# A routed expert layer whose first rows come in three transfers, and whose row numbers are moved later

## The chip, the cores and the metric

The kernel runs on one core of one Trainium2 chip. The metric is device time in microseconds (us) of one execution. All engines named here belong to that core: TensorE (PE), VectorE (DVE), ScalarE (ACT), GpSimd (POOL) and SyncE (SP), with 16 DMA engines that all queues share.

## The reference

Three steps follow one another, all in 32-bit floats. First an attention with a decaying state over 768 positions gives 3072 tokens of 384 channels. Then each token goes to the one of 8 experts that its logits pick. Then every token goes through one dense layer pair.

```
x = attention(r, k, v, w, u)                      # (3072, 384)
logits = x @ w_gate; e = argmax(logits)           # one of 8 experts
x[e] = gate * (relu(x[e] @ w1[e]) @ w2[e])        # 384 -> 1024 -> 384
h = x @ w_in; out = max(0.01 * h, h) @ w_out      # 384 -> 2048 -> 384
```

## The kernel before

**Routing.** While the attention runs, POOL scatters finished rows, each of 384 channels and a 385th column with the token's own number, into `x_rows` in DRAM, where every expert has its own region. When the last tile is routed, DVE works out a table of groups: each group is 416 rows of one expert. In the profiled execution there are 8 groups. `grouped` is the semaphore that says the tables are there.

**One group (stage of the experts).** `load_x(n)` (ACT's DMA queue, L1199) brings the 416 rows of group n as 104 partitions x 4 rows x 385 numbers. PE turns them with 12 transposes (L1081), three tiles of columns `d` by four blocks. ACT copies each tile to `x_hi` (L1215), rounded to the matmul's format, and DVE takes the rest, `x_lo` (L1274). Each of 8 hidden blocks `f` is 9 matmuls (L1098: 3 tiles by hi*hi, lo*hi, hi*lo), then a relu by ACT into `h_hi` (L1220) and its rest by DVE into `h_lo` (L1281). Each block goes into the output through 9 more matmuls (L1114), two blocks behind the hidden ones: PE's order in a group is 12 transposes, output blocks 6 and 7 of the group before, hidden 0, 1, 2, output 0, hidden 3, output 1, and so on. The first hidden matmul waits for `parts_ready` of the group's w1, and output block 0 for that of its w2.

**ACT's order in a group.** Three `x_hi` copies, `load_x(n + 1)`, `move_ids(n)`, then the eight relus. `move_ids(n)` (L1208) copies the 416 token numbers of the group, 4 bytes each, from column 385 of `x_rows` to `id_rows` in DRAM. Both read their addresses from the group tables with register loads (L998).

**Weights.** SP loads an expert's weights in seven pieces (three of w1 with 128 x 1024 numbers, four of w2 with 128 x 768) into a `stage` of two halves (L116). Piece m is issued when the split of piece m-2 is done. POOL splits each piece into `w_hi` (L130) and `w_lo` (L134), and small `tick` instructions (L120) carry its waits in the loop. Group 0's weights are ready before the stage begins. The pieces of group 1 are issued once the first rows have landed (SP waits for `x_loaded`). The pieces of w_in and w_out follow those of the last group.

**After the groups.** DVE splits the first dense input (L1297, L1300), PE goes through six dense groups (L1153, L1174), and POOL scatters the results by the numbers from `id_rows`.

Of the kernel before, what the change touches and what calls it, by code (L numbers as in the profile page):

```python
# [13 lines left out]
def build_program(nc, r, k, v, wu, moe_w_gate, moe_w1, moe_w2, moe2_w_in, moe2_w_out, out):  # L14
    C, HP, _, DH, B, P = r.shape
# [9 lines left out]
    DC = D // P  # L25
# [11 lines left out]
    U = 416  # L37
    TR = U // 4
# [8 lines left out]
    x_rows = nc.dram_tensor("x_rows", (E * RR, XW), F32, kind="Internal").ap()  # L47
    id_rows = nc.dram_tensor("id_rows", (N + U, 1), F32, kind="Internal").ap()

    def expert_pieces(e):  # L50
        w1e = moe_w1[e:e + 1] if isinstance(e, int) else moe_w1[bass.ds(e, 1)]
        w2e = moe_w2[e:e + 1] if isinstance(e, int) else moe_w2[bass.ds(e, 1)]
        p = [(c * FE, FE, w1e[:, c * P:(c + 1) * P, :].rearrange("o p f -> p o f")) for c in range(DC)]
        p += [(DC * FE + f * D, 2 * D, w2e[:, f * P:(f + 2) * P, :].rearrange("o (f p) d -> p (o f) d", p=P))
              for f in range(0, FC, 2)]
        return p
# [15 lines left out]
    with ctx:  # L72
        def sb(name, shape, dt=F32, stack=ctx):
            return stack.enter_context(nc.sbuf_tensor(name, shape, dt))
# [4 lines left out]
        def sem(name, stack=ctx):  # L79
            return stack.enter_context(nc.semaphore(name))  # L80
# [858 lines left out]
        def layers():  # L939
# [3 lines left out]
            rows = sb("rows", [P, G, XW], stack=st2)  # L943
# [14 lines left out]
            ps_o = bank[2:6]  # L958


            x_loaded = sem("x_loaded")
            ids_moved = sem("ids_moved")
            xt_mm = sem("xt_mm")
# [32 lines left out]
            def entry(eng, table, n, most):  # L996
                at = table[0:1, n:n + 1] if isinstance(n, int) else table[0:1, bass.ds(n, 1)]
                return eng.value_load(at, min_val=0, max_val=most)  # L998

            def on_sync(sp):  # L1000
                def weights(n, b):
                    e = entry(sp, group_e, n, E - 1)
                    for i, piece in enumerate(expert_pieces(e)):
                        issue_piece(sp, n * NPE + i, (b * NPE + i) % 2, piece)

                sp.wait_ge(grouped, 1)
                pairs, last = pairs_of(sp), last_of(sp)


                sp.wait_ge(x_loaded, 16)  # L1010
                weights(1, 1)
                with sp.Fori(1, pairs) as t:
                    for b in range(2):
                        weights(t * 2 + b, b)
                base = last * NPE + NPE
                for n, piece in enumerate(w_in_pieces()):
                    issue_piece(sp, base + n, n % 2, piece)
                base = base + NPI
                for n, piece in enumerate(w_out_pieces()):
                    issue_piece(sp, base + n, n % 2, piece)  # L1020

                sp.wait_ge(stored, STORES * NG)
# [52 lines left out]
            def on_tensor(pe):  # L1075
                def transposes(n):

                    pe.wait_ge(x_loaded, n * 16 + 16)
                    for d in range(DC):
                        for t in range(4):  # L1080
                            i = pe.transpose(ps_x[d][:, t * TR:(t + 1) * TR], rows[0:TR, t, d * P:(d + 1) * P],  # L1081
                                             ident[0:TR, 0:TR])
                        i.then_inc(xt_mm, 1)
# [47 lines left out]
                pairs, last = pairs_of(pe), last_of(pe)  # L1131
# [61 lines left out]
            def on_scalar(act):  # L1193
                def load_x(n):
                    row = entry(act, group_row, n, E * RR - U)
                    if isinstance(n, int) and n == 0:
                        act.wait_ge(filled, 16 * ZEROS)
                        act.wait_ge(scattered, SCATTERS * C)
                    act.dma_start(rows[0:TR, :, :],  # L1199
                                  x_rows[bass.ds(row, U), :].rearrange("(t p) d -> p t d", p=TR)).then_inc(x_loaded, 16)  # L1200

                def move_ids(n):


                    row, off = entry(act, group_row, n, E * RR - U), entry(act, group_off, n, N)
                    if not isinstance(n, int) or n > 0:
                        act.wait_ge(ids_moved, n * 16)
                    act.dma_start(id_rows[bass.ds(off, U), :], x_rows[bass.ds(row, U), D:D + 1],  # L1208
                                  allow_slow_non_contiguous=True).then_inc(ids_moved, 16)

                def group(n, b):
                    for d in range(DC):

                        act.wait_ge(xt_mm, n * DC + (d + 1))
                        act.activation(x_hi[:, b, d, 0:U], ps_x[d][:, 0:U], ACT.Copy).then_inc(xt_hi_ok, 1)  # L1215
                    load_x(n + 1)
                    move_ids(n)
                    for f in range(FC):
                        act.wait_ge(h_mm, n * FC + (f + 1))
                        act.activation(h_hi[:, f % NB, 0:U], ps_h[f % 2][:, 0:U], ACT.Relu).then_inc(h_hi_ok, 1)  # L1220

                act.wait_ge(grouped, 1)
                pairs = pairs_of(act)
                load_x(0)
                group(0, 0)
                group(1, 1)
                with act.Fori(1, pairs) as t:
                    group(t * 2, 0)
                    group(t * 2 + 1, 1)

                act.wait_ge(ids_moved, pairs * 32)
                act.dma_start(ids_f[:, :].unsqueeze(2), id_rows[U:N + U, :].rearrange("(m p) o -> p m o", p=P),
                              allow_slow_non_contiguous=True).then_inc(ids_in, 16)

                def dense(g, first=False):
                    for f in range(FFC + 1):
                        if f < FFC:

                            act.wait_ge(d_mm, g * FFC + (f + 1))
                            act.activation(hc[:, f % 2, :], ps_h[f % 2][:, :], ACT.Copy).then_inc(d_ok, 1)  # L1240
                        if f >= 1:

                            act.wait_ge(g_ok, g * FFC + f)
                            act.activation(h_hi[:, (f - 1) % NB, :], gf[:, (f - 1) % 2, :], ACT.Copy).then_inc(gh_ok, 1)  # L1244
                    if first:

                        act.wait_ge(x_loaded, pairs * 32 + 16)
                    else:

                        act.wait_ge(stored, g * STORES)  # L1250
                    for t in range(2):
                        act.wait_ge(o_mm, g * G + (t + 1))
                        act.activation(rows[:, t, 0:D], ps_o[t][:, 0:D], ACT.Copy).then_inc(o_act, 1)  # L1253

                dense(0, True)
                with act.Fori(1, NG) as g:
                    dense(g)

            def on_vector(dve):
# [26 lines left out]
                pairs, last = pairs_of(dve), last_of(dve)  # L1286
# [21 lines left out]
                def dense(g, b, more=True):  # L1308
                    for f in range(FFC):

                        dve.wait_ge(d_ok, g * FFC + (f + 1))
                        if not (isinstance(g, int) and g == 0 and f < 2):
                            dve.wait_ge(gh_ok, g * FFC + (f - 1))

                        dve.scalar_tensor_tensor(gf[:, f % 2, :], ps_h[f % 2][:, :], 0.01, hc[:, f % 2, :],  # L1315
                                                 ALU.mult, ALU.max).then_inc(g_ok, 1)
                        dve.wait_ge(gh_ok, g * FFC + (f + 1))
                        dve.tensor_tensor(h_lo[:, f % NB, :], gf[:, f % 2, :], h_hi[:, f % NB, :].bitcast(F32),  # L1318
                                          ALU.subtract).then_inc(gl_ok, 1)
                        if more and f == MID:  # L1320
                            x_split(g + 1, 1 - b)
                        if isinstance(g, int) and g == 0 and f == MID:

                            dve.wait_ge(ids_in, 16)
                            dve.tensor_copy(ids_i[:, :], ids_f[:, :]).then_inc(ids_ok, 1)
                    if not (isinstance(g, int) and g == 0):
                        dve.wait_ge(stored, g * STORES)
                    else:
                        dve.wait_ge(x_loaded, pairs * 32 + 16)
                    for t in range(2, G):  # L1330
                        dve.wait_ge(o_mm, g * G + (t + 1))
                        dve.tensor_copy(rows[:, t, 0:D], ps_o[t][:, 0:D]).then_inc(o_dve, 1)
# [68 lines left out]
```

## Time and profile before

| | us |
|---|---|
| median of 3 runs | 831.3 |
| lowest, highest | 830.53, 842.6 |
| profiled execution, its own time | 825.21 |
| span of the profiled execution | 823.5 |
| PE busy | 771.5 (94%) |
| DVE, ACT, POOL busy | 335.7, 215.1, 335.3 |

The span is what the trace covers, and all places in it below are counted from its start. The attention and the routing end at about 164 us, the groups run from 166 to about 403 us, and the dense layers fill the rest.

### The profile page before, as it was taken

To read this page: it belongs to the slowest core of one execution; us is meant where nothing else is said; L and a number is where in the kernel's file an instruction comes from. 1 tells how busy PE (TensorE), PEld (TensorE's weight loads), DVE (VectorE), ACT (ScalarE), POOL (GpSimd) and SP (SyncE) were. 2 spreads that over 40 slices of the span, in tenths; PEclk is the share of its full clock that TensorE was granted. 3 is DMA by queue.
4 is the path that set the end of the run, shared out by engine and by line. 5 is a ranking of instruction groups with operands and counts; after the bars stand their busy time and mean duration, and the time that the engine had idled before them with its cause. 6 is when DMAs were issued, how large, how long until landed. Compare 5 with 4: busy or idle time off the path is not lost.

```text
span 823.5 us, 17748 instructions
## 1 busy us (share of the span) xinstructions
PE 771.5 (94%) x7200; PEld 707.7 (86%) x7200; DVE 335.7 (41%) x658; ACT 215.1 (26%) x436; POOL 335.3 (41%) x338
## 2 busy tenths in 40 slices
PE   9889889469998989999899999999999999999995
PEld 8778777459998989999889889989988998998994
DVE  7868755613233133223544333433433433433332
ACT  2224433311122112111122232222232223232221
POOL 6568855637767677976991010010010001001001
PEclk9999989779999999999999999999999999999998
DMA  4757654354665355356430000010000000001000
GB/s 145 225 159 208 182 164 148 117 125 136 109 124 150 91 146 157 103 146 146 115 117 1 1 38 1 1 39 1 1 38 0 0 0 38 0 0 39 1 1 39
DMA packets 42611, 66.91 MB, mean 81 GB/s; under 512 B 11413, under 2 KB 31797, under 8 KB 42549
## 3 DMA queue, kind: packets, MB, share of 16 engines
q1 hardware_dynamic: 28944, 50.76, 22.6%
q10 hardware_dynamic: 10533, 5.80, 3.7%
q0 software_dynamic: 3072, 9.45, 3.1%
q8 instruction: 47, 0.77, 0.4%
q14 instruction: 15, 0.12, 0.1%
HBM read 51.42 MB, written 14.59 MB: 80 GB/s over the span
## 4 chain that ended last, share of the span: by engine, by line
PE 79%; POOL 9%; issue 5%; DMA 3%; DVE 2%; ACT 0%; ACTq 0%; POOLq 0%; SPq 0%; DVEq 0%
PE bank L1174 24%; PE bank L1153 24%; PE bank L1114 7%; PE bank L1098 7%; POOL w_lo L134 5%; PE ps_y L833 3%; POOL w_hi L130 2%; DMA stage<-in_moe_w 2%; PE ps_y L818 2%; PE ps_x L790 2%; PE ps_s L770 2%; PE ps_x L786 2%; PE ps_l L854 1%; PE ps_x L845 1%; PE ps_m L804 1%
## 5 line engine op out<-in xcount | busy, mean ns | idle before, releaser
L1042 POOL DMA_INDIRECT out_rows<-rows,ids_i x24 | 23.1, 962 | 358.7 <-ACT rows L1253 353.2
L1318 DVE TENSOR_TENSOR h_lo<-gf,h_hi 128x512 fp32r<-128x512 f32 x96 | 70.2, 732 | 227.4 <-ACT h_hi L1244 227.4
L134 POOL TENSOR_TENSOR w_lo<-stage,w_hi 128x768 fp32r<-128x768 f32 (+1 forms) x70 | 146.4, 2092 | 5.8
L1174 PE MATMUL bank<-w_hi,h_hi 128*128 128x384 f32 x384 | 130.4, 339 | 0.0
L1174 PE MATMUL bank<-w_lo,h_hi 128*128 128x384 f32 x384 | 129.3, 337 | 0.0
L1174 PE MATMUL bank<-w_hi,h_lo 128*128 128x384 f32 x384 | 129.1, 336 | 0.0
L1240 ACT ACTIVATE hc<-bank 128x512 f32<-128x512 f32 x96 | 57.4, 597 | 273.1 <-PE bank L1153 273.1
L1153 PE MATMUL bank<-x_hi,w_hi 128*128 128x512 f32 x288 | 114.0, 396 | 2.3 <-DVE x_lo L1300 2.3
L1153 PE MATMUL bank<-x_lo,w_hi 128*128 128x512 f32 x288 | 114.3, 397 | 0.0
L1153 PE MATMUL bank<-x_hi,w_lo 128*128 128x512 f32 x288 | 113.9, 395 | 0.0
L1281 DVE SCALAR_TENSOR_TENSOR h_lo<-bank,h_hi 128x416 fp32r<-128x416 f32 x64 | 37.7, 591 | 149.5 <-ACT h_hi L1220 149.5
L1220 ACT ACTIVATE h_hi<-bank 128x416 fp32r<-128x416 f32 x64 | 33.0, 517 | 174.2 <-PE bank L1098 170.7
L1174 PEld LDWEIGHTS bank<-w_hi,h_hi 128*128 128x128 f32 x384 | 72.1, 188 | 6.9 <-issue 3.3
L1174 PEld LDWEIGHTS bank<-w_hi,h_lo 128*128 128x128 f32 x384 | 72.2, 188 | 3.5
L130 POOL TENSOR_SCALAR w_hi<-stage 128x768 fp32r<-128x768 f32 (+1 forms) x70 | 65.4, 934 | 20.3 <-DMA stage<-in_moe_w 20.1
L1114 PE MATMUL bank<-h_hi,w_hi 128*128 128x416 f32 x192 | 68.4, 356 | 4.5 <-POOLq L140 4.5
L1174 PEld LDWEIGHTS bank<-w_lo,h_hi 128*128 128x128 f32 x384 | 72.2, 188 | 0.0
L1315 DVE SCALAR_TENSOR_TENSOR gf<-bank,hc 128x512 f32<-128x512 f32 x96 | 65.6, 683 | 11.2 <-ACT hc L1240 11.2
L1098 PE MATMUL bank<-x_hi,w_hi 128*128 128x416 f32 x192 | 68.0, 354 | 0.8 <-DVE h_lo L1281 0.8
L1114 PE MATMUL bank<-h_lo,w_hi 128*128 128x416 f32 x192 | 67.7, 353 | 0.0
L1098 PE MATMUL bank<-x_hi,w_lo 128*128 128x416 f32 x192 | 67.7, 352 | 0.0
L1114 PE MATMUL bank<-h_hi,w_lo 128*128 128x416 f32 x192 | 67.6, 352 | 0.0
(170 smaller groups left out, 1185.5 us busy)
## 6 DMA issues: line engine op xcount, KB each, us to landing
stage<-in_moe_w SPq DMA_DIRECT2D x24, 512.0 KB, 6.0
stage<-in_moe_w SPq DMA_DIRECT2D x32, 384.0 KB, 3.1
rows<-x_rows ACTq DMA_DIRECT2D x9, 625.6 KB
x_rows<-pad_row SPq DMA_DIRECT2D x32, 156.4 KB
k_u<-in_k SPq DMA_DIRECT2D x48, 96.0 KB, 3.0
r_u<-in_r SPq DMA_DIRECT2D x48, 96.0 KB, 2.7
v_u<-in_v SPq DMA_DIRECT2D x24, 192.0 KB, 3.5
stage<-in_moe_w_in SPq DMA_DIRECT2D x6, 512.0 KB, 4.3
```

The costliest lines, as they stand in the source:

```text
L130: eng.tensor_scalar(w_hi[:, buf, off:off + cols], stage[:, h, 0:cols], 1.0, 0.0, ALU.mult, ALU.add).then_inc(split_hi, 1)
L134: i = eng.tensor_tensor(w_lo[:, buf, off:off + cols], stage[:, h, 0:cols], w_hi[:, buf, off:off + cols].bitcast(F32), ALU.subtract)
L833: ins = pe.matmul(ps_y[halves[j], t, b * L:(b + 1) * L], am[halves[j], g % 2, t, b, :], v_cols(i, j, t, b, L), start=False, stop=True, ski ...
L1098: i = pe.matmul(ps_h[f % 2][:, 0:U], ww[:, b, o:o + P], x[:, b, d, 0:U], start=d == 0 and ww is w_hi and x is x_hi, stop=d == DC - 1 and x ...
L1114: i = pe.matmul(ps_y[d][:, 0:U], ww[:, b, o:o + P], h[:, f % NB, 0:U], start=f == 0 and ww is w_hi and h is h_hi, stop=f == FC - 1 and h i ...
L1153: i = pe.matmul(ps_h[f % 2][:, :], ww[:, 0, o:o + P], x[:, b, d, :], start=d == 0 and ww is w_hi and x is x_hi, stop=d == DC - 1 and x is ...
L1174: i = pe.matmul(ps_o[t][:, 0:D], x[:, f % NB, t * P:(t + 1) * P], ww[:, 1, o:o + D], start=f == 0 and x is h_hi and ww is w_hi, stop=f == ...
L1220: act.activation(h_hi[:, f % NB, 0:U], ps_h[f % 2][:, 0:U], ACT.Relu).then_inc(h_hi_ok, 1)
L1240: act.activation(hc[:, f % 2, :], ps_h[f % 2][:, :], ACT.Copy).then_inc(d_ok, 1)
L1281: dve.scalar_tensor_tensor(h_lo[:, f % NB, 0:U], ps_h[f % 2][:, 0:U], 0.0, h_hi[:, f % NB, 0:U].bitcast(F32), ALU.max, ALU.subtract).then_ ...
L1315: dve.scalar_tensor_tensor(gf[:, f % 2, :], ps_h[f % 2][:, :], 0.01, hc[:, f % 2, :], ALU.mult, ALU.max).then_inc(g_ok, 1)
L1318: dve.tensor_tensor(h_lo[:, f % NB, :], gf[:, f % 2, :], h_hi[:, f % NB, :].bitcast(F32), ALU.subtract).then_inc(gl_ok, 1)
```

## The change

The load of group 0 becomes three DMAs, one for each tile of 128 columns, each with its own semaphore `x_first[d]`; the number column isn't loaded for this group. The four transposes of tile `d` wait for `x_first[d]` alone. SP waits for the last of the three. All later loads stay whole, and their counts on `x_loaded` are one load lower. In every group `move_ids(n)` goes from ahead of the relus to behind the second of them.

```diff
@@ on_sync
-                sp.wait_ge(x_loaded, 16)
+                sp.wait_ge(x_first[DC - 1], 16)
                 weights(1, 1)
@@ on_tensor, transposes(n)
-                    pe.wait_ge(x_loaded, n * 16 + 16)
+                    if not isinstance(n, int) or n > 0:
+                        pe.wait_ge(x_loaded, n * 16)
                     for d in range(DC):
+                        if isinstance(n, int) and n == 0:
+                            pe.wait_ge(x_first[d], 16)
                         for t in range(4):
@@ on_scalar, load_x(n)
-                    act.dma_start(rows[0:TR, :, :],
-                                  x_rows[bass.ds(row, U), :].rearrange("(t p) d -> p t d", p=TR)).then_inc(x_loaded, 16)
+                        for d in range(DC):
+                            cols = slice(d * P, (d + 1) * P)
+                            act.dma_start(rows[0:TR, :, cols], x_rows[bass.ds(row, U), cols]
+                                          .rearrange("(t p) d -> p t d", p=TR)).then_inc(x_first[d], 16)
+                    else:
+                        act.dma_start(rows[0:TR, :, :], x_rows[bass.ds(row, U), :]
+                                      .rearrange("(t p) d -> p t d", p=TR)).then_inc(x_loaded, 16)
@@ on_scalar, group(n, b)
                     load_x(n + 1)
-                    move_ids(n)
                     for f in range(FC):
+                        if f == 2:
+                            move_ids(n)
                         act.wait_ge(h_mm, n * FC + (f + 1))
                         act.activation(h_hi[:, f % NB, 0:U], ps_h[f % 2][:, 0:U], ACT.Relu).then_inc(h_hi_ok, 1)
```

ACT's instructions from the first load on stand so before:

```order
L1199 DMA rows<-x_rows 104x4x385
L1215 ACTIVATE x_hi<-bank 128x416 [waits xt_mm] x3
...
L1199 DMA rows<-x_rows 104x4x385
...
L1208 DMA id_rows<-x_rows 416x1
L1220 ACTIVATE h_hi<-bank 128x416 [waits h_mm] x8
```

and so after the change:

```order
L1206 DMA rows<-x_rows 104x4x128
L1206 ISA
L1206 DMA rows<-x_rows 104x4x128
L1206 ISA
L1206 DMA rows<-x_rows 104x4x128
L1225 ACTIVATE x_hi<-bank 128x416 [waits xt_mm] x3
...
L1209 DMA rows<-x_rows 104x4x385
L1231 ACTIVATE h_hi<-bank 128x416 [waits h_mm] x2
...
L1218 DMA id_rows<-x_rows 416x1
L1231 ACTIVATE h_hi<-bank 128x416 [waits h_mm] x6
```

The copy of the numbers and the register loads in front of it moved from ahead of eight relus to between the second and the third.

## Rows read from the trace of the kernel before

**Rows 1.** The page: busy time, and TensorE's clock in 40 slices.

```profile
PE 771.5 (94%) x7200; PEld 707.7 (86%) x7200; DVE 335.7 (41%) x658; ACT 215.1 (26%) x436; POOL 335.3 (41%) x338
PEclk9999989779999999999999999999999999999998
```

**Rows 2.** The chain that ended last: start, length, what.

```profile
165.89 5.88 DMA rows<-x_rows
...
180.08 8.15 DMA stage<-in_moe_w
...
299.79 0.46 PE bank L1114
```

**Rows 3.** Stretches of one group each: length, busy times, clock, DMA share, GB/s.

```profile
199.80:227.80 28.00, 28.00 (x159) 27.94 (x157) 8.02 (x14) 5.47 (x11) 20.93 (x20) 1.00 0.64 136
...
256.00:288.00 32.00, 29.89 (x159) 29.35 (x158) 8.05 (x14) 5.47 (x11) 21.96 (x24) 0.95 0.51 119
288.00:319.30 31.30, 28.95 (x160) 27.94 (x159) 8.04 (x14) 5.47 (x11) 25.88 (x27) 1.00 0.47 134
319.30:347.30 28.00, 28.00 (x159) 27.95 (x158) 8.04 (x14) 5.47 (x11) 22.55 (x25) 1.00 0.50 137
```

**Rows 4.** Timeline of PE and ACT at the first group: start, length, engine, what.

```profile
171.81 2.34 PE L1081 MATMUL bank<-ident,rows 104*128 104x104 f32 x12 [15.59 <-DMA rows<-x_rows]
174.09 0.68 PE L1098 MATMUL bank<-x_hi,w_hi 128*128 128x416 f32 x1
179.38 0.45 PE L1098 MATMUL bank<-x_hi,w_hi 128*128 128x416 f32 x1 [0.81 <-DVE h_lo L1281]
...
175.33 0.58 ACTq L1199 DMA_DIRECT2D rows<-x_rows  x1
177.44 0.69 ACTq L1208 DMA_DIRECT2D id_rows<-x_rows  x1
178.18 0.93 ACT L1220 ACTIVATE h_hi<-bank 128x416 fp32r<-128x416 f32 x2 [3.48 <-issue]
```

**Rows 5.** Timeline of POOL, ticks, with the idle time before each.

```profile
205.27 0.44 POOL L120 TENSOR_TENSOR tick<-tick 128x1 f32<-128x1 f32 x2 [0.35 <-POOL w_lo L134]
214.11 0.19 POOL L120 TENSOR_TENSOR tick<-tick 128x1 f32<-128x1 f32 x1 [4.91 <-DMA stage<-in_moe_w]
...
241.06 0.19 POOL L120 TENSOR_TENSOR tick<-tick 128x1 f32<-128x1 f32 x1 [3.48 <-DMA stage<-in_moe_w]
...
264.62 0.19 POOL L120 TENSOR_TENSOR tick<-tick 128x1 f32<-128x1 f32 x1 [3.05 <-DMA stage<-in_moe_w]
...
380.43 0.19 POOL L120 TENSOR_TENSOR tick<-tick 128x1 f32<-128x1 f32 x1 [0.39 <-POOL w_lo L134]
```

**Rows 6.** Waits from 172 to 410 us: total, times, longest.

```profile
POOL tick L120 <- DMA stage<-in_moe_w: 33.6, 19, 4.9
...
PE bank L1114 <- POOLq L140: 4.5, 2, 2.4
```

**Rows 7.** The moves of the numbers: landing after issue (L1208), and ACT in group 1.

```profile
DMA to landing us min/median/max: 8.0/9.0/10.8
...
203.72 0.56 ACTq L1208 DMA_DIRECT2D id_rows<-x_rows  x1
...
207.67 0.52 ACT L1220 ACTIVATE h_hi<-bank 128x416 fp32r<-128x416 f32 x1 [1.16 <-PE bank L1098]
```

**Rows 8.** Two stretches with PE's busy time: length, busy, clock, DMA share, GB/s.

```profile
187.00:189.00 2.00, 2.00 (x12) 1.00 0.73 271
...
209.00:213.20 4.20, 4.20 (x24) 1.00 0.79 53
```

**Rows 9.** DMA queues at 166.5:171, 173:177, 218:228: packets, MB, share; weight landing.

```profile
q10 hardware_dynamic: 429, 0.64, 68.3%
q1 hardware_dynamic: 274, 1.02, 67.0%
q1 hardware_dynamic: 816, 1.18, 38.4%
...
stage<-in_moe_w SPq DMA_DIRECT2D x4, 384.0 KB, 3.1
```

**Rows 10.** DVE's split of the first dense input, same shape.

```profile
405.10 0.42 DVE L1297 TENSOR_SCALAR x_hi<-z_t 128x512 fp32r<-128x512 f32 x1
...
406.88 2.59 DVE L1297 TENSOR_SCALAR x_hi<-z_t 128x512 fp32r<-128x512 f32 x1
```

More of the change, by code:

```diff
@@ L958, in layers @@
             ps_o = bank[2:6]
+            x_first = [sem(f"x_first{d}") for d in range(DC)]
             x_loaded = sem("x_loaded")
@@ L1245, in dense @@
                     if first:
-                        act.wait_ge(x_loaded, pairs * 32 + 16)
+                        act.wait_ge(x_loaded, pairs * 32)
                     else:
@@ L1328, in dense @@
                     else:
-                        dve.wait_ge(x_loaded, pairs * 32 + 16)
+                        dve.wait_ge(x_loaded, pairs * 32)
                     for t in range(2, G):
```

## The prediction

> **What bounds the kernel now.** I read the page first. PE is busy for 94% of the span, and its clock falls only in the slices from about 144 to 185 us, where routing ends and the groups start [rows 1]. So time is to be had only around that start, or where PE waits later. The chain of waits shows who owns the start: it runs through the first rows' load (5.88 us), then through a weight piece and POOL, and back to PE only at 299.79 [rows 2]. The windows by group say what that costs. A group takes 28.0 us where PE never waits, but 32.0 and 31.3 in two of them [rows 3], so 7.3 us are lost there. Of these 4.5 are PE waiting for w2 of the group to be split (L1114 behind POOL) [rows 6], and the rest is the restart at a lower or unsettled pace. From 319 us on PE never waits in the groups.
>
> Why is POOL late? From the start of group 2's weights (205.27) to the end of group 7's (380.43) it needs 175.2 us [rows 5], 29.2 per group. It waits for stage DMAs 33.6 us [rows 6], 5.6 per group, which leaves 23.6 of work. PE's pace of 28.0 thus leaves room for 28.0 - 23.6 = 4.4 us of DMA waits a group, and 5.6 are spent.
>
> Who makes these DMAs slow? Four w2 pieces in a quiet stretch land 3.1 us after issue [rows 9], but one w1 piece took 8.15 [rows 2]. It was issued at 180.08, just behind a move of the row numbers (177.44 [rows 4]). Behind the next such move (203.72 [rows 7]) the DMA engines are 79% busy at 53 GB/s, where they otherwise reach 271 at 73% [rows 8], and POOL waits 4.91 [rows 5]. A move lands 8.0 to 10.8 us after issue (median 9.0) [rows 7]. I call that stretch the hole. The first load of rows in a group slows pieces too, less.
>
> The Trainium skill (DMA: Bandwidth & Descriptors, Specifications) says that transfers under 512 B are done as read-modify-write. The trace agrees as far as it shows 4-byte copies with a hole behind them; it doesn't show the cause.
>
> **The change, part by part.**
>
> *Three loads for one.* The three DMAs are issued 0.58 us each [rows 4] plus about 0.08 between them, so the last at 165.89 + 2 x 0.66 = 167.2 instead of 165.89. There are three times the packets, each a third as long: 96 instead of 32 on each of 13 engines (104 partitions). No row has a 512-byte packet. Two rows of weights give 0.670 x 4 x 16 / 274 = 156 ns for 3.7 KB and 0.384 x 10 x 16 / 816 = 75 ns for 1.45 KB [rows 9], a line that gives 42 ns at 512 B and 79 at 1540. The old load took 0.683 x 4.5 x 16 / 429 = 115 ns a packet [rows 9], or 3.7 us in all. New: 96 x 42 = 4.0 us (line) or 96 x 61 = 5.9 (line, scaled by 115/79); the far end is 96 x 115 = 11.0, if the price goes by packet. I take the line and a little of the scaling: the last rows land at 172.3 instead of 171.8 (ends 171.0 and 179).
>
> The skill (same page, Rules for kernel authors) wants many small transfers coalesced, which speaks against this edit. By the overhead of three cycles per packet that the page gives (Why small descriptors are slow), 512 B would cost 19 beats instead of 16, some 10% more in all, an estimate of +0.4 us; the sum above doesn't use it.
>
> *Earlier transposes.* 12 transposes take 2.34 us at half clock, and the first matmul follows at 174.09 [rows 4]. Eight of them, and their copies, now run before the last rows land, so the matmul follows the landing by 0.8 instead of 2.3: 1.5 gained, minus 0.5 for the later landing, 1.0. SP's first weight piece goes 0.5 later.
>
> *The numbers behind relu 1, group 0.* Relu 0 started 3.48 late behind register loads and DMA issues, and PE stood 0.81 at 179.38 for its rest h_lo, with 0.2 of restart [rows 4]. With the move behind it, relu 0 runs when its block is done: 1.0 gained. Queued behind the move now are relus 2 to 7. The move costs ACT 1.5 of register loads (175.91 to 177.44) and 0.7 of issue [rows 4], so relu 2 is up to 1 us late; PE asks for its result only at hidden 4, after output 0, hidden 3 and output 1, over 5 us later. Cost nothing; if that cover were gone, 1 us in each group.
>
> *The numbers, later groups.* The move goes out after relu 1 (207.67 + 0.52) and 1.6 of loads, at 209.8 instead of 203.7 [rows 7], 6 us later. PE had no stall there, so PE gains nothing. SP and POOL are the ones touched: the hole now starts 8 us behind the load of rows, not 2, and falls on w1 pieces of the next group instead of the last w2 and first w1. Before, both slow stretches often joined; now POOL meets two, and each is covered by what it has staged (one piece being split, one landed, about 3.3 us each). Bounds of the DMA wait per group: 2.8 (each is covered by a piece more) and 7.9 (a wait as at 264.62, 3.05, and one as at 214.11, 4.91 [rows 5]). I take 5.2, near the 5.6 of now, since the moves' bytes are the same and only the queueing behind the rows goes.
>
> **Sum.** PE reaches group 1 2.0 us earlier. The weights of group 1 are ready at 205.2 and PE asks for them at 199.8 + 9.5 = 209.3 (12 transposes, five blocks), a lead of 4.1 that shrinks to 2.1. Excess over the room is 5.2 - 4.4 = 0.8 in each of six groups, 4.8, minus the lead: 2.7 of waits and some 1.3 of restarts, 4.0, where 7.5 were lost (7.3 and 0.2 in a third group). So 3.5 + 2.0 = 5.5 faster: 825.2 - 5.5 = 819.7 in an execution like the profiled one. That one lies 6.1 under the median of the runs shown (831.3), and the number to be compared is such a median: 831.3 - 5.5 = 826. The same check on the kernel before (1.2 x 6 - 4.1 = 3.1) gives less than the 4.5 seen, so the tally is good to some 2 us.
>
> One term is set to nothing for lack of a sign: DVE's split before the dense layers, where an instruction took 0.42 or 2.59 [rows 10], as it seems by what POOL does beside it. With three of them, -4 to +2 us.
>
> **Rivals.**
> - *PE-bound throughout.* If the DMA wait per group is under 4.75, the lead covers it and all 7.5 go: -9.5, 822. For it: the holes no longer join, so POOL's stock counts twice. Against: both holes remain.
> - *Nothing.* The waits for w2 eat what PE gained at the start, since POOL's clock starts with the last rows, as late as before: within 2 us, 831. For it: the chain runs through POOL until 299.79.
> - *Slower: two holes, two waits.* Place: POOL's stage in each group. With 7.9 of DMA wait the excess is 3.5 x 6 - 2.1 = 19 of PE waits and 4.5 of restarts, against 7.5 now and 2.0 gained: +14, 845. It decides from about 6.0 per group, where waits and restarts reach 9.5. For it: the move now goes out just as SP issues w1 pieces, the largest, and a load of rows alone already made a wait of 3.05. Against: in group 4 to 6 of the profile, where POOL was least disturbed, one hole cost 3.5 or less.
> - *The loads cost by packet.* Last rows at 179: everything behind is up to 7 later, less 2.5 gained: +5, 836.
>
> **How the numbers follow.** Forecast (2 to 8 us faster) 0.40, PE-bound 0.15, nothing (within 2) 0.20, two waits 0.17, by packet 0.08. The likeliest gives 826. The range goes from just beyond PE-bound with a good DVE split, 818, to half of the two-wait case, 838. A measurement of this kernel tells about 2%, 16.6 us, from no change. Faster than that takes PE-bound and a luckier split together, 0.03; slower takes the far end of the two-wait case with slow loads, 0.04; within, 0.93.
>
> **What would show it.** Last rows landing near 172.3, first matmul 0.8 behind, no PE stall for h_lo of block 0, the moves near 210 in group 1, POOL's waits for stage near 5.2 a group, PE's waits behind POOL (4.5 now) under 3. Waits of PE in every group would mean the two-wait case; none at all the PE-bound one. The forecast is wrong if the hole is caused by something other than the moves of the numbers.

## The result, and the profile after

| | before | changed |
|---|---|---|
| median | 831.54 us | 849.28 us |
| lowest, highest (4 runs each) | 830.53, 842.6 | 847.29, 858.78 |
| ratio, 95% interval | | 1.020, 1.0136 to 1.0264 |
| profiled execution, own time | 825.21 | 851.05 |
| span | 823.5 | 849.3 |

The change made the kernel 17.7 us slower. Forecast were 826 us and a range up to 838, so the prediction was wrong in sign and outside its range. The slower rival, "two holes, two waits", had stood at 845. Each ratio here and below compares only runs in the faster of a kernel's two states, while medians take in all runs.

All places below are from the start of their own kernel's span. The changed kernel's chain of waits, as start, length and what, answers to [rows 2]:

```profile
175.12 4.34 DMA rows<-x_rows
180.19 3.68 DMA stage<-in_moe_w
187.67 11.29 DMA stage<-in_moe_w
203.09 2.95 DMA stage<-in_moe_w
209.05 6.05 DMA stage<-in_moe_w
```

The first rows are no slower, but the weight piece that took 8.15 us before now takes 11.29, and one more of 6.05 has joined the chain.

The start itself went as intended. This is PE's timeline at the first group, to be read against [rows 4]:

```profile
177.06 0.96 PE L1086 MATMUL bank<-ident,rows 104*128 104x104 f32 x4 [12.88 <-DMA rows<-x_rows]
178.81 1.65 PE L1086 MATMUL bank<-ident,rows 104*128 104x104 f32 x8 [0.80 <-DMA rows<-x_rows]
180.16 0.69 PE L1103 MATMUL bank<-x_hi,w_hi 128*128 128x416 f32 x1
```

The first load is issued at 173.85, so the first matmul comes 6.3 us behind it, where it was 174.09 - 165.89 = 8.2. The wait of 0.81 for `h_lo` is gone (PE has no such wait in a second profile of the kernel before either). Now the same stretch from the first transpose of group 1 to that of group 7, six groups (length, then busy times with their counts, PE's clock, DMA share, GB/s), of the kernel before:

```profile
199.65:374.99 175.34, 170.88 (x938) 168.85 (x937) 48.23 (x84) 32.84 (x66) 134.16 (x138) 0.99 0.53 130
```

and of the changed kernel, with its groups 1 and 3 alone:

```profile
205.98:397.27 191.29, 175.48 (x938) 171.45 (x937) 48.27 (x84) 32.86 (x66) 135.47 (x138) 0.97 0.51 120
205.98:237.22 31.24, 28.88 (x157) 27.89 (x156) 8.03 (x14) 5.48 (x11) 22.20 (x22) 1.00 0.57 122
269.12:301.17 32.05, 29.87 (x158) 29.31 (x156) 8.05 (x14) 5.47 (x11) 22.75 (x24) 0.95 0.50 119
```

Six groups without a wait are 6 x 28.0 = 168. The kernel before needed 175.3, the changed one 191.3, and here lie 16 us of the loss. The waits say the same; these are the changed kernel's, from 172 to 430 us, to be read against [rows 6]:

```profile
POOL tick L120 <- DMA stage<-in_moe_w: 45.9, 18, 5.2
...
PE bank L1119 <- POOLq L140: 15.8, 6, 3.6
```

PE waits for w2 in six groups instead of two (in one, for 2.3 us, in the second profile of the kernel before). POOL's timeline shows the pattern, two waits in nearly every group, to be read against [rows 5]:

```profile
226.33 0.20 POOL L120 TENSOR_TENSOR tick<-tick 128x1 f32<-128x1 f32 x1 [4.24 <-DMA stage<-in_moe_w]
...
246.92 0.19 POOL L120 TENSOR_TENSOR tick<-tick 128x1 f32<-128x1 f32 x1 [3.95 <-DMA stage<-in_moe_w]
...
258.26 0.20 POOL L120 TENSOR_TENSOR tick<-tick 128x1 f32<-128x1 f32 x1 [4.36 <-DMA stage<-in_moe_w]
...
277.98 0.19 POOL L120 TENSOR_TENSOR tick<-tick 128x1 f32<-128x1 f32 x1 [2.93 <-DMA stage<-in_moe_w]
...
289.97 0.20 POOL L120 TENSOR_TENSOR tick<-tick 128x1 f32<-128x1 f32 x1 [4.79 <-DMA stage<-in_moe_w]
```

The waits of 2.9 to 4.0 are for the last w2 piece, slowed by the load of the next rows (issued at 239.28 and 271.17). Those of 4.2 to 4.8 are for a w1 piece behind the move of the numbers. That move is now issued 9.5 us into group 1 instead of 4.1:

```profile
215.49 0.56 ACTq L1218 DMA_DIRECT2D id_rows<-x_rows  x1
```

Its landing is somewhat shorter in the median, 8.2 us against 9.0 [rows 7], but the hole behind it is as deep as before [rows 8]:

```profile
216.70:222.00 5.30, 4.00 (x21) 3.90 (x22) 0.54 (x1) 0.24 (x1) 4.86 (x5) 1.00 0.63 23
```

The DMA engines are 63% busy at 23 GB/s there. Outside the groups, 8.0 us of the 25.8 between the two spans come before the first load, where both kernels run the same code, and are not the change's. From the first load to group 1's transposes the changed kernel is 1.6 us shorter, in the six groups 16.0 longer, and from group 7's transposes to the end 3.5 longer (452.0 against 448.5). These three make 17.8, close to the 17.7 between the medians. Between the profiles of 14 executions the first load's issue lay anywhere from 162.9 to 184.3 us; the four latest, from 176.8 on, are the four of one chip. Medians over several executions are compared for that reason, and from profiles mainly the stretches inside the groups.

### The profile page after: what moved, and what is told of

It reads as the page before. It is cut to its first block, busy times and chain, and to the rows that moved or that the text cites. A ratio compares the mean times of both kernels' runs of the same rounds, so it can differ in the third digit from the quotient of the medians.

```text
span 849.3 us, 17753 instructions
## 1 busy us (share of the span) xinstructions
PE 784.2 (92%) x7200; PEld 715.8 (84%) x7200; DVE 340.3 (40%) x658; ACT 215.5 (25%) x436; POOL 335.9 (40%) x338
## 4 chain that ended last, share of the span: by engine, by line
PE 69%; POOL 14%; issue 8%; DMA 3%; DVE 3%; another core or an unknown queue 1%; ACT 0%; ACTq 0%; POOLq 0%; SPq 0%; DVEq 0%
PE bank L1179 24%; PE bank L1158 23%; POOL w_lo L134 9%; POOL w_hi L130 4%; PE ps_y L833 4%; DMA stage<-in_moe_w 3%; PE bank L1119 3%; PE bank L1103 3%; PE ps_y L818 2%; PE ps_x L790 2%; PE ps_s L770 2%; PE ps_x L786 1%; PE ps_m L804 1%; PE ps_l L854 1%; PE ps_x L845 1%
## 5 line engine op out<-in xcount | busy, mean ns | idle before, releaser
L1119 PE MATMUL bank<-h_hi,w_hi 128*128 128x416 f32 x192 | 69.6, 363 | 15.8 <-POOLq L140 15.8
```

The costliest lines, as they stand in the source:

```text
L1119: i = pe.matmul(ps_y[d][:, 0:U], ww[:, b, o:o + P], h[:, f % NB, 0:U], start=f == 0 and ww is w_hi and h is h_hi, stop=f == FC - 1 and h i ...
```

## The experiments

Ratios are to runs of the kernel before on the same chip in the same series (medians 833.07, 818.47 and 818.45 us for the three series). "Six groups" is the stretch from the first transpose of group 1 to that of group 7, from each kernel's own profile, "first" the time from the first load's issue to the first hidden matmul.

| kernel | median us | ratio (95%) | first | six groups |
|---|---|---|---|---|
| before | | | 8.2 | 175.3 |
| before, again | 826.52 (one run) | | 8.1 | 173.5 |
| changed | 849.28 | 1.020 (1.014 to 1.026) | 6.3 | 191.3 |
| changed, again | 835.52 | 1.020 (1.012 to 1.029) | 6.6 | 188.0 |
| three loads alone | 839.13 | 1.007 (1.000 to 1.014) | 6.3 | 173.6 |
| numbers behind relu 1 alone | 849.62 | 1.025 (1.017 to 1.033) | 8.4 | 182.0 |
| numbers behind relu 5 | 849.59 | 1.022 (1.012 to 1.031) | 8.3 | 181.7 |
| numbers ahead of next rows | 863.38 | 1.037 (1.026 to 1.047) | 8.1 | 200.7 |
| second copy, DRAM to DRAM | 861.33 | 1.051 (1.040 to 1.062) | 8.2 | 209.9 |
| second copy, DRAM to SBUF | 825.3 | 1.011 (1.002 to 1.019) | 8.1 | 167.9 |
| long rows | 829.03 | 1.015 (1.005 to 1.026) | 8.0 | 176.3 |
| long rows, short numbers | 816.72 | 0.997 (0.994 to 1.001) | 7.9 | 167.9 |
| changed, short numbers | 816.32 | 0.999 (0.995 to 1.002) | 7.8 | 168.8 |
| one load, late, short numbers | 816.52 | 1.000 (0.996 to 1.004) | 7.7 | 168.8 |

### Each half of the change alone

```diff
 three loads alone (against the changed kernel)
                     load_x(n + 1)
+                    move_ids(n)
                     for f in range(FC):
-                        if f == 2:
-                            move_ids(n)
 numbers behind relu 1 alone (against the kernel before)
                     load_x(n + 1)
-                    move_ids(n)
                     for f in range(FC):
+                        if f == 2:
+                            move_ids(n)
```

> The three loads alone; the numbers are moved where they were before, ahead of the relus. Theory A (the loss of 17.7 us comes from where the hole behind the move of the numbers falls, so that POOL meets two slow stretches a group): this kernel stands with the one before, 831.5, or 1 to 2 us under it, and PE waits for w2 behind POOL about 4 to 6 us in all. Theory B (the three loads or their later landing cost it): 840 or more, with group 1's weights late from the start.

> The move of the numbers behind relu 1 alone; the first rows come in one load. Theory A: all of the loss, 846 to 851, PE waits 2 to 4 us for w2 in each of groups 1 to 6, POOL waits for stage DMAs over 7 us a group. Theory B: 828 to 833.

The loss is in the second half: 1.025, with four waits of PE behind POOL (10.3 us) in its profile, not one in each of six groups as expected. Its six groups are 182.0 us, 9.3 shorter than those of the whole change, though its ratio is no lower. Against the three loads alone, on the same chip, 8.4 us of its 14.2 lie in the six groups and 6.8 behind them, so the loss isn't confined to the six groups. The three loads have six groups like those before (173.6) and a first matmul 1.9 us sooner. Their ratio of 1.007 is still barely above one, and not the gain of 1 to 2 us that theory A left room for. Its ten runs spread from 828.75 to 851.6, and from the first load on its profile is 4.5 us shorter than the one before (653.1 against 657.6). The stretch up to the first load, the same code in both, is 14.3 us longer, but no profile of the kernel before was taken on that chip, so where those 7 parts in a thousand lie stays open.

### Other places for the move

```diff
 numbers behind relu 5: as behind relu 1, with
+                        if f == 6:
 numbers ahead of next rows
+                    move_ids(n)
                     load_x(n + 1)
-                    move_ids(n)
```

> One load; the numbers are moved behind relu 5, some 20 us into a group. Theory A, two slow stretches far apart are what costs: the hole now ends as the next load of rows starts, the two join again, and the time is 826 to 834. Rival A2 (any place later than the old one costs, because the hole falls on pieces that POOL needs and ACT's queue gets later): 845 or more. If relus stall behind the register loads, PE shows waits for h_lo.

> One load; the numbers are moved just ahead of the next rows' load instead of just behind. Theory A: the slow stretches still join, 828 to 835. The move no longer queues behind the rows' packets, so its landing should fall from a median of 9.0 to 7.5 or 8 us. Rival A3 (it is the order on ACT's queue that matters, the rows then crawl through the hole): rows land over 10 us after issue and the time rises to 840 or more.

Both times my theory A failed, and the rivals written beside it (A2, 845 or more; A3, 840 or more) had the times right. I had taken joined slow stretches for cheap wherever they lie. Ahead of the next rows they join, and it is the worst of the places tried: POOL's waits of 3 to 5 us become single ones of over 8, and PE waits 27.2 us in three waits. This is POOL's timeline:

```profile
229.69 0.20 POOL L120 TENSOR_TENSOR tick<-tick 128x1 f32<-128x1 f32 x1 [8.34 <-DMA stage<-in_moe_w]
...
256.70 0.19 POOL L120 TENSOR_TENSOR tick<-tick 128x1 f32<-128x1 f32 x1 [9.44 <-DMA stage<-in_moe_w]
```

The median landing of the move itself stayed at 8.8 us instead of falling to 7.5 or 8. Behind relu 5, too, hole and rows come close together, and POOL's longest waits are 5.7 to 7.6. What both have in common, as I read it, is that the load of 640 KB now has to pass through the hole, and the weight pieces queue with it. At the old place the rows are issued 2 us ahead. In group 1 of the kernel before all their 0.64 MB move between 203.7 and 208 us, ahead of the hole at 209 [rows 8]. So the rule is not "keep the two together" but "the move behind the rows, at once". These two kernels bear on its first half; its second rests on the numbers behind relu 1, some 6 us later than the old place and 2.5% slower.

### What makes the hole

```diff
 second copy (against the kernel before), behind relu 1
+                        if f == 2:
+                            again(n)
 to DRAM
+                    act.dma_start(spare[bass.ds(off, U), :], x_rows[bass.ds(row, U), D:D + 1], ...)
 or to SBUF
+                    act.dma_start(spare_s[0:TR, :].unsqueeze(2), x_rows[bass.ds(row, U), D:D + 1]
+                                  .rearrange("(t p) o -> p t o", p=TR), ...)
```

> The kernel before, with a second copy of the same 416 numbers, DRAM to DRAM into a spare tensor, issued behind relu 1 of each group (the first stays where it was). Theory C (a 4-byte move DRAM to DRAM by itself stops the other DMAs for some 7 us, whatever else is in flight): POOL waits over 9 us a group, the group stage (238 us from the first transposes to the first dense matmul) grows by 25 us or more, 855 to 875. Rival (the old place was a hole because two transfers of ACT's queue met): under 845.

> The same, but the second copy reads the 416 numbers from DRAM into a spare SBUF tile: 416 packets of 4 bytes as well, without a write to DRAM. Theory C1 (the writes of 4 bytes to DRAM make the hole): 828 to 838, its landing 2 to 4 us after issue. Theory C2 (the scattered 4-byte reads or the number of packets make it): as the second write, 855 or more, landing 7 us or later.

Both copies read the same 416 numbers in packets of 4 bytes from the same place; the profiles count 14,869 and 14,846 packets under 512 bytes, against 11,413 before. The one that writes them to DRAM costs 5.1%. In its profile POOL waits 65.1 us, and PE 31.4 in three waits; these are its lines:

```profile
POOL tick L122 <- DMA stage<-in_moe_w: 65.1, 23, 7.2
...
PE bank L1117 <- POOLq L142: 31.4, 3, 12.0
```

The copy into SBUF leaves the six groups with no PE wait at all, and costs 1.1%, or nothing that its profile shows in the groups:

```profile
199.09:367.01 167.92, 167.92 (x937) 167.58 (x936) 48.23 (x84) 32.84 (x66) 133.50 (x137) 1.00 0.53 134
```

It is the 4-byte writes to DRAM, then, not the reads or the number of packets. Whether it matters that both ends lie in DRAM was not tried: no copy of long pieces from DRAM to DRAM was run. That profile also holds the old hole of each group without one PE wait, which shows how narrow the margin is on which the kernel before stands.

### Taking the hole away

```diff
 long rows (against the kernel before)
-  x_rows[bass.ds(row, U), :].rearrange("(t p) d -> p t d", p=TR)
+  x_rows[bass.ds(row, U), :].rearrange("(p t) d -> p t d", p=TR)
-  pe.transpose(ps_x[d][:, t * TR:(t + 1) * TR], rows[0:TR, t, ...
+  pe.transpose(ps_x[d][:, 0:U].rearrange("p (c t) -> p c t", t=4)[:, :, t], rows[0:TR, t, ...
 short numbers
+  act.activation(ids_s[0:TR, b, :].unsqueeze(2), rows[0:TR, 0:4, D:D + 1], ACT.Copy).then_inc(ids_kept, 1)
+  act.wait_ge(ids_kept, n + 1)      # ahead of load_x(n + 1)
-  act.dma_start(id_rows[bass.ds(off, U), :], x_rows[bass.ds(row, U), D:D + 1], ...)
+  act.dma_start(id_rows[bass.ds(off, U), :].rearrange("(p t) o -> p (t o)", p=TR), ids_s[0:TR, b, :])
```

> Only the rows in runs of 6,160 bytes and the transposes with a stride of four; the numbers are moved as before, 4 bytes DRAM to DRAM. Theory C1: the hole stays, the load of rows slows pieces less, and the time is 824 to 832. Rival (the load of rows is the disturbance that matters): as the long runs of both, 818 to 826. The first rows should land 1 to 2 us earlier than 5.9 after issue.

> Each partition takes four rows that follow one another (one run of 6,160 bytes instead of four of 1,540), the transposes write every fourth column so that the tokens keep their order, and the numbers go from a small SBUF copy to DRAM in runs of 16 bytes, 104 packets instead of 416, at the old place in the order. Theory C1: fewer writes, a hole of 2 to 3 us instead of 7; POOL waits under 4.4 us a group, PE never waits for w2, and the group stage falls from 238 to 226 to 232: 818 to 826. Rival (the hole is a fixed cost of any small copy behind the rows): 828 to 835. If transposes with a stride of four are slower in PE, each group gets up to 1 us longer.

The longer runs of the rows alone do nothing for the hole (six groups 176.3 with one PE wait of 5.9, ratio 1.015), and the first matmul comes 0.2 us sooner, not 1 to 2, against what I expected. With the numbers in 104 writes of 16 bytes no hole shows. The profile doesn't give the landing of this move. It is issued at 207.88 in group 1, and most of its packets run between 212 and 214 us, where the DMA engines move 289 GB/s at 90% busy, against 53 at 79% behind the old move [rows 8]. PE waits for w2 nowhere:

```profile
212.00:214.00 2.00, 2.00 (x13) 2.00 (x12) 0.59 (x1) 0.55 (x2) 0.40 (x2) 1.00 0.90 289
...
POOL tick L120 <- DMA stage<-in_moe_w: 21.6, 17, 4.3
```

Over six groups POOL's waits stay inside the room that PE's pace leaves. The same edit was then put under the change:

> The changed kernel (three first loads, numbers behind relu 1) with the hole taken away: four following rows to a partition, and the numbers go from a small SBUF copy in 104 runs of 16 bytes. Theory A with C1 (the place costs only because the writes of 4 bytes make a hole): PE never waits for w2, steps between groups 28.0 us, group stage 228 to 232 us, and the time lies with the long runs at the old place or up to 2 us under it, 18 us or more under the change. Rival (the place itself costs, by ACT's queue or by relus held up): over the kernel before by 10 us or more.

> As the one before, but the first rows come in one load: only the numbers are late, and short. Theory A with C1: no PE wait for h_lo of block 0 (0.8 us before), else equal to the version with three loads within 2 us, which shows what the three loads alone are worth where nothing hides them (1.0 us forecast, at most 1.5).

> The changed kernel once more, on this chip. Theory A says that its two slow stretches bind whatever the chip: 1.5 to 4% slower than the kernel before, PE waits for w2 in most of the groups, group stage 250 to 258 us. If the loss were a matter of the first chip, the two would be equal here.

> The kernel before once more, for a second profile of it. If the start of the groups' first load (165.9 us in its profile, 163 to 184 in the others, whose code up to there is the same) is a matter of the execution, it moves by several us here as well. The group stage should be 230 (PE never waits) to 240 us.

The changed kernel with short numbers, six groups:

```profile
196.32:365.16 168.84, 168.84 (x937) 167.62 (x936) 48.28 (x84) 33.42 (x72) 138.58 (x143) 1.00 0.50 141
```

Its POOL waits 14.1 us for w1 and w2 pieces where the change itself, on the same chip, waits 42.7. The move sits as late as in the change, and the loss is gone: 0.999 against 1.020 in the same series. So this place costs only through the hole. This is also the answer to the rival that blamed ACT's queue. The changed kernel again gave the same ratio on another chip:

```profile
196.66:384.68 188.02, 172.34 (x938) 168.62 (x936) 48.25 (x84) 32.85 (x66) 135.56 (x138) 0.99 0.52 122
```

No version beats the kernel before beyond its interval. On the chips of the last two series its median is 818.5, with 816.3 to 816.7 for the three versions with short numbers. Their ten runs each span 8 to 11 us, those of the kernel before 15 (13 runs) and 23 (19 runs).

## Why the prediction was wrong

**The start: right for the first matmul, and larger there.** Forecast were 1.0 us from earlier transposes (last rows 0.5 later) and 1.0 from relu 0. The first matmul came 1.9 us sooner in the change's profile and in the three loads alone, 1.6 in the second profile of the change. SP's first weight piece shows the last rows to have landed 5.6 us after the first issue, not 6.4: 512-byte packets cost less than the line through two longer sorts gave. (The low end of 171.0 given for that landing doesn't follow from this line: 96 x 42 ns behind the 2.2 us that the old load took beside its packets gives 172.1.) PE's stall for `h_lo` went. Group 1 starts 32.1 us behind the first load instead of 33.8, so 1.6 of the 2.0 arrived. The 1.0 for relu 0 is not borne out: with the late numbers alone the stall is gone too, yet group 1 starts 33.9 us behind the first load. From 9.5 to 11.5 us behind that load PE's granted clock is 0.69 there and 0.86 in the kernel before, so the full clock came later. With three 512-byte loads on top of the (p t) order of rows nothing was gained (first 7.8 against 7.7 with one load). The profile shows what took the gain away:

```profile
162.85 3.54 ACTq L1208 DMA_DIRECT2D rows<-x_rows  x3
...
165.55 4.38 DMA rows<-x_rows
```

ACT needs 3.54 us to issue the three, where it needed 1.60 in the change. The last one goes out 2.7 us behind the first instead of 1.3, and lands 4.38 later, as in the change (4.34). Why these issues take longer no run shows.

**The numbers, later groups: the step that failed.** I put POOL's DMA wait at 5.2 us a group. From 218.25, the first tick of group 2's weights, to 405.13, the one behind group 7's, POOL took 186.9 us with 45.9 of waits: 7.6 a group, beside 23.5 of work. The bounds I had given were 2.8 and 7.9, and the true value lay at the end that I called the two-wait case. The reason that I gave for the lower value, that POOL's staged pieces cover each stretch separately, is what the timeline refutes: a wait of 2.9 to 4.0 for the last w2 piece (five times) and one of 3.7 to 5.2 for the second w1 piece (six times). The move is issued 9.5 to 9.7 us into a group, just when SP issues the next w1 pieces, and the ticks show POOL waiting after the split of a single w1 piece: it had one piece in stock and not two.

**The lead: not seen.** I let the lead of 4.1 us shrink by PE's gain alone. But group 0's own move now goes out 6.6 us behind its first weight piece instead of 5.0 (186.79 - 180.19, 177.44 - 172.49), with a third w1 piece issued 0.9 behind it that takes 11.29 us, and the last w2 piece meets the next load of rows (6.05). The weights of group 1 were ready at 218.0, 44.1 us behind the first load, instead of 39.3; PE asked for them at 215.6. The lead was -2.4.

With 7.6 and -2.4 the prediction's own tally reads 3.2 x 6 + 2.4 = 21.6 of waits, and the trace has 15.8 of waits and 7.5 of slower pace and clock behind them: 191.3 - 168 = 23.3. The tally's 21.6 is thus near the whole loss, but not near the waits, and the prediction would have added restarts to it. Its error is small beside that of the value fed to it. On the evidence of the profile before, the two-wait case deserved more than 0.17. There were waits of 3.0 to 3.4 for the rows' load and of 3.1 to 4.9 for the moves. In group 2 of the kernel before both stood one behind the other, this one for the rows' load and the one of 3.48 at 241.06 [rows 5] for the move:

```profile
234.20 0.19 POOL L120 TENSOR_TENSOR tick<-tick 128x1 f32<-128x1 f32 x1 [3.37 <-DMA stage<-in_moe_w]
```

That is 6.9 us in one group already, above the 6.0 from which the prediction itself saw the slower rival decide.

**The cause of the hole: right.** That the moves of the numbers make it was the prediction's assumption, and the second copy into DRAM bears it out: one more such copy adds its own waits, and with the writes made longer they go. The Trainium skill's sentence that transfers under 512 B are done as read-modify-write (DMA: Bandwidth & Descriptors, Specifications) agrees with the two second copies as far as it concerns writes: 4 bytes to DRAM stop the others, 4 bytes to SBUF don't. Why 16-byte writes are so much lighter no run separates, since their number fell to a quarter too and their source became SBUF.

**The rest.** The row of the clock shows a fall to 0.8 in the slice from 103 to 124 us too [rows 1], which the prediction passed over; it lies in the attention, which the change leaves alone. The term set to nothing, DVE's split before the dense layers, went the wrong way. In the changed kernel two of its three roundings took 2.6 us beside POOL's work, where one did before [rows 10], and PE waited 1.98 once more. They are a part of the 3.5 us lost from group 7's transposes to the end. These are the two:

```profile
427.74 2.60 DVE L1308 TENSOR_SCALAR x_hi<-z_t 128x512 fp32r<-128x512 f32 x1
...
431.86 2.58 DVE L1308 TENSOR_SCALAR x_hi<-z_t 128x512 fp32r<-128x512 f32 x1
```

## What to carry to other kernels

A transfer's price is also what it does to the others in flight: a copy of 1.6 KB that nobody waits for decided here whether PE waited in two groups or in six. Before moving such a copy, mark what each other queue has in flight at the new place, and add the waits instead of counting on stock to cover each. Where a stage has as little room as POOL's here (4.4 us of 28.0 for all its DMA waits), cure the disturbing transfer (fewer and longer writes) rather than its place; once it was cured, the place no longer mattered.

## What the runs showed of the hardware

- 416 writes of 4 bytes, DRAM to DRAM, take 7.9 to 9.2 us to land in the median (12.3 for a second copy issued 5.5 us behind the first), and for 4 to 5 of these the other transfers crawl (23 and 53 GB/s at 63 and 79% busy). The profile's packets of the move are over before that: in the change's group 1 the last 244 run between 217 and 218 us, and the slow stretch lasts to 222. The same 416 numbers copied into SBUF beside an unchanged move cost PE no wait. From SBUF in 104 runs of 16 bytes no slow stretch follows (289 GB/s at 90% busy while they run).
- Transposes into every fourth column of PSUM cost PE nothing that shows: 2.34 us for the first twelve at half clock in either form, as the version with long rows and short numbers has it:

```profile
176.48 2.34 PE L1083 MATMUL bank<-ident,rows 104*128 104x104 f32 x12 [15.16 <-DMA rows<-x_rows]
```

- Behind many of its waits PE ran the rest of the group some 3.5% slower at a granted clock of 1.00. A wait is not needed for it: group 1 of both late kernels with short numbers takes 28.9 us so, without one. ACT's idle time before a relu is 2.96 us there against 2.84 elsewhere, as in the changed kernel's group 1:

```profile
225.24 0.52 ACT L1231 ACTIVATE h_hi<-bank 128x416 fp32r<-128x416 f32 x1 [2.96 <-PE bank L1103]
```

  It makes 0.9 us a group (31.24 - 2.36 - 28.0), and nothing in these profiles says why. In three of the change's six groups the granted clock is 0.95 as well, and 1.7 to 1.9 us are lost beside the wait.
